# High parts of the MLP's weights cast on ScalarE, and the tail's constant products placed anew, in a kernel of attention and two mixtures

## The chip, the cores and the metric

One core of a Trainium2 chip runs the whole kernel. The metric is the device time of one execution in microseconds (us); lower is better. The result is compared with a reference in float32.

## The reference, cut to what matters

Three stages follow each other: causal attention with a decay (4 batches, 8 heads, 576 tokens, head size 64), an MLP with the gate h * sigmoid(1.702 h) (512 to 2048 to 512, on 2304 tokens), and a soft mixture of 8 experts over 32 slots.

```python
# attention
scores = scale * np.matmul(q, k.transpose(0, 1, 3, 2))
scores = np.where(causal, -1000000000.0, scores + decay)
attn = softmax(scores)                    # rows, with the maximum taken off
x = attn @ v                              # to (B*S, H*D)
# MLP
h = x @ w_in
x = (h * (1.0 / (1.0 + np.exp(-1.702 * h)))) @ w_out
# soft mixture
logits = x @ phi                          # 2304 x 32
d = exp(logits - logits.max(0)); d /= d.sum(0) + 1e-09
slot_input = d.T @ x                      # 32 x 512, over all tokens
slot_out[e] = np.maximum(slot_input[e] @ w1[e], 0.0) @ w2[e]
c = exp(logits - logits.max(1)); c /= c.sum(1) + 1e-09
out = c @ slot_out
```

## The kernel before, in words

Five engines run programs of their own that meet at semaphores: TensorE (PE) multiplies, VectorE (DVE), ScalarE (ACT) and GpSimd (POOL) move, split and scale, SyncE (SP) issues every DMA. Each runs its own instructions strictly in the order of the program text, so a wait holds back all that stands behind it on that engine.

**Split products.** A product of two float32 matrices is made of three faster ones: each operand is split into a high part (rounded to fp32r) and a low part (what is left), and PE multiplies high by high, high by low and low by high. For the MLP's weights, SP loads a piece of 128x512 into one of two slots of `stage` (`load_w`, L497), VectorE casts it into `wih` or `woh` (`w_split`, L790), and GpSimd subtracts the high part from the staged piece into `wil` or `wol` (L660). The next piece for that slot is loaded only when GpSimd has finished. There are 128 pieces: 4 batches, 4 quarters of the hidden size, 4 pieces of `w_in` and 4 of `w_out` each.

**Order.** `batch_steps` writes out one list of steps for each engine. Batch 0 of attention (to about 98 us) runs alone; then the heads of batches 1 to 3 are interleaved with the MLP of the batch before (to about 583 us), the MLP of the last batch runs alone (to about 696 us), and the tail with the experts follows. Batch 0's own four casts of the first quarter are steps of their own (`("split", t)`).

**MLP units.** An MLP of a batch has 64 units of 12 matmuls of 288 columns. In each quarter the first 8 units (kind 0) make hidden values: ScalarE takes the tanh out of PE's bank (`gate`, L729), VectorE makes `hid` from it and frees the bank (L921), ScalarE casts `hid` of the unit before to `gh` (L723), GpSimd makes `gl` (L643). The second 8 units (kind 1) multiply by `w_out`; VectorE adds the bank to `x2t` (L926, L928), ScalarE has no work but the last `gh`. PE alternates between two banks of `mb`, so a unit starts only when the bank of the unit before last has been read. VectorE's cast of piece t stands behind its own work of units 0, 1, 3 and 4 of a kind (`SPLIT_AT`): the pieces of `w_out` in kind 0, those of the next quarter's `w_in` in kind 1.

**A batch's last head.** The last head of a batch is finished in the next batch's first slot: ScalarE copies `olow` (L702), VectorE adds `xst` (L844), ScalarE casts `xh` (L706), VectorE subtracts `xl` (L849), and the next MLP may begin.

**Tail.** The logits of the last batch are turned (L1148, L1149), VectorE takes the maximum over tokens (`gmax`, L943), PE turns it (L1216), VectorE reduces it (`smax`) and makes a diagonal (`dmax`), PE spreads that to all partitions (L1220), VectorE subtracts it (`ew`, L950), ScalarE takes the exponential (L743), and PE sums tokens into slots (`dispatch`, L1231, 40 matmuls of 512 columns). `busy(n)` issues n matmuls of constants (L1159), whose results nobody reads. Then come the 8 experts. Their weights, 16 loads of 2 MB, go through a ring of ten buffers: the load of the tenth buffer (`ring_x`, L504) is issued when the dispatch is done (third count of `t_pe`), and the six loads that reuse a buffer when the expert before has been computed.

Of the kernel before, what the change touches and what calls it, by code (L numbers as in the profile page):

```python
# [53 lines left out]
SPLIT_AT = (0, 1, 3, 4)  # L54
# [12 lines left out]
TURN_AT = 6  # L67
SOFTMAX_AT = (8, 9, 10, 11, 18, 19, 20, 21)
SOFTMAX_EXP = 13
BUSY = (7, 16)  # L70
INV_SQRT_D = DIM ** -0.5
MASKED = 1e9
GATE = 1.702
# [159 lines left out]
def build(nc, q, k, v, f, w_in, w_out, phi, w1, w2, out):  # L233
    ctx = ExitStack()
    with ctx:
# [239 lines left out]
        def w_pieces(u, last):  # L475

            c, kind, j = unit_kind(u)
            if kind == 0:
                return c, 4, c
            if kind == 1 and not (last and c == QUARTERS - 1):  # L480
                return c + 1, 0, (c + 1) % QUARTERS
            return None
# [185 lines left out]
        def _(act):  # L668
            act.wait_ge(f_clip, 1)
            nc.scalar.activation(logf, f_sb, ACT.Ln).then_inc(f_log, 1)  # L670

            def step(b, m, st):
                if st[0] == "qk":
                    par = st[1] % 2
# [23 lines left out]
                elif st[0] == "pv":  # L698
                    s = st[1]
                    r0 = 64 * (s % 2)  # L700
                    act.wait_ge(attended, b * 8 + s + 1)
                    nc.scalar.copy(olow[r0:r0 + 64, :], pv_ps[64:P, :]).then_inc(o_low, 1)  # L702
                elif st[0] == "xsplit":
                    kt = st[1]
                    act.wait_ge(o_sum, m * 8 + 2 * kt + 2)
                    nc.scalar.copy(xh[:, kt, :], xst[:, kt, :]).then_inc(x_hi, 1)  # L706
                elif st[0] == "post":
                    for i in LAST_POST[st[1]]:
                        act.wait_ge(post_token, m * QT + i + 1)
                        nc.scalar.copy(x2last[0:QW[i], i, :], last_tokens[i][0:QW[i], :]).then_inc(token_out, 1)  # L710
                elif st[0] == "token":
                    i = st[1]
                    r = QW[i]
                    act.wait_ge(post_token, m * QT + i + 1)
                    nc.scalar.copy(x2tok[0:r, m * QT + i, :], bank_of("token", m, i)[0:r, :]).then_inc(token_out, 1)
                elif st[0] == "unit":
                    u = st[1]
                    c, kind, j = unit_kind(u)
                    k1 = m * 32 + 8 * c

                    def high(i):
                        act.wait_ge(unit_out, m * U_MLP + 16 * c + i + 3)
                        nc.scalar.copy(gh[:, i % FT, HALF * (i // FT):HALF * (i // FT + 1)],  # L723
                                       hid[:, i % RING, :]).then_inc(g_hi, 1)

                    if kind == 0:
                        act.wait_ge(unit_done, m * U_MLP + u + 1)
                        act.wait_ge(g_lo, k1 + j + 1)
                        nc.scalar.activation(gate[:, j % RING, :], bank_of("unit", m, u)[:, 0:HALF], ACT.Tanh,  # L729
                                             scale=GATE / 2).then_inc(h_tanh, 1)  # L730
                        if j:
                            high(j - 1)
                    elif j == 0:
                        high(7)
                    if m and u == SOFTMAX_EXP:
                        act.wait_ge(c_dve, (m - 1) * C_CHAIN + 2)
                        nc.scalar.activation(e5[:, :, :], e5[:, :, :], ACT.Exp).then_inc(c_exp, 1)
# [30 lines left out]
        def _(dve):  # L768
# [14 lines left out]
            dve.wait_ge(f_log, 1)  # L783
            dve.wait_ge(pads_made, 1)
            nc.vector.tensor_tensor_scan(cum, one_row, logf, 0.0, ALU.mult, ALU.add).then_inc(cum_made, 1)

            def w_split(order, which, t):
                hi = (wih, woh)[which]
                dve.wait_ge(w_dma[t % 2], 16 * ((order >> 1) + 1) if isinstance(order, int) else (order - t % 2) * 8 + 16)
                nc.vector.tensor_copy(hi[:, t, :], stage[:, t % 2, :]).then_inc(w_hi, 1)  # L790

            def step(b, m, st):
                if st[0] == "qk":
# [52 lines left out]
                elif st[0] == "xsplit":  # L846
# [1 line left out]
                    dve.wait_ge(x_hi, m * 4 + kt + 1)  # L848
                    nc.vector.tensor_tensor(xl[:, kt, :], xst[:, kt, :], xh[:, kt, :].bitcast(F32),  # L849
                                            ALU.subtract).then_inc(x_lo, 1)  # L850
                elif st[0] == "split":
                    w_split(st[1], 0, st[1])
                elif st[0] == "logits":
                    dve.wait_ge(post_logits, m + 1)
                    keep_turned(bank_of("logits", m, 0))
# [55 lines left out]
            def unit(b, m, u):  # L911
# [11 lines left out]
                else:  # L923
# [3 lines left out]
                    else:  # L927
                        nc.vector.scalar_tensor_tensor(out=dst, in0=bank[:, 0:HALF], scalar=0.5, in1=dst,  # L928
                                                       op0=ALU.mult, op1=ALU.add).then_inc(unit_out, 1)
                pieces = w_pieces(u, last)  # L930
                if pieces and j in SPLIT_AT:
                    t = SPLIT_AT.index(j)
                    w_split(m * 32 + 8 * pieces[0] + pieces[1] + t, pieces[1] // 4, t)
                if m and u in SOFTMAX_AT:
                    (keep_maxima, keep_values, token_max, token_sub, token_sum, token_eps, token_inv, token_weights
                     )[SOFTMAX_AT.index(u)](m - 1)
# [85 lines left out]
        def _(pe):  # L1022
# [188 lines left out]

            pe.wait_ge(lt_made, 1 + BATCH)
            turn_logits(last_turn)
            pe.wait_ge(t_dve, 1)
            pe.wait_ge(token_out, 1 + (BATCH - 1) * QT + 2)
            tr(zb[0:SLOTS, 0, 0:P], gmax[:, :], ident[:, :]).then_inc(t_pe, 1)  # L1216
            turn_last(4)
            busy(BUSY[0])
            pe.wait_ge(t_dve, 3)
            mm(zb[:, 1, 0:SLOTS], ones[0:SLOTS, :], dmax[:, :], start=True, stop=True).then_inc(t_pe, 1)  # L1220
            busy(BUSY[1])
            pe.wait_ge(t_act, 1)
            pe.wait_ge(t_dve, 4)
            pe.wait_ge(token_out, 1 + BATCH * QT)
# [107 lines left out]
```

## Time and profile before

| | us |
|---|---|
| median of 3 runs | 772.56 |
| lowest, highest | 771.88, 776.73 |
| the profiled execution's own time | 776.32 |
| its span, first to last instruction | 774.5 |
| PE busy | 718.1 |
| VectorE busy | 495.7 |
| GpSimd busy | 411.4 |
| ScalarE busy | 370.8 |

The profiled execution is 3.8 us longer than the median of the unprofiled runs, and lies near the highest of them. Its time is its span and 1.8 us around it. A busy time says how long an engine had an instruction in work; PE's matmuls overlap, so a busy PE isn't one at its peak. What counts for the time is where PE, the engine that is busy almost throughout, stood idle or ran at the lower clock.

### The profile page before, as it was taken

Reading aid. Unit: us, or ns where it says so; the run is one execution under the profiler, and the core shown is the slowest. Engines: PE = TensorE matmul, PEld = TensorE weight load, DVE = VectorE, ACT = ScalarE, POOL = GpSimd, SP = SyncE. Lnnn points to the kernel's source line nnn. Section 1 sums busy time; section 2 is a strip of 40 time slices with the busy share of each in tenths; the row PEclk is TensorE's granted clock in tenths of the full one; section 3 lists DMA queues with packets and bytes.
Section 4 is the critical chain, followed back from the end, with each engine's and each line's share of the span. In section 5 each row is a group of like instructions: output and inputs, shape, how many; then the busy total and the mean of one; then the engine's idle time right before and its main releaser. Section 6 shows DMA issues by size and latency. Waiting matters only on the chain.

```text
span 774.5 us, 15770 instructions
## 1 busy us (share of the span) xinstructions
PE 718.1 (93%) x6024; PEld 680.7 (88%) x6024; DVE 495.7 (64%) x1383; ACT 370.8 (48%) x903; POOL 411.4 (53%) x439
## 2 busy tenths in 40 slices
PE   3999979999999898999999989999999999998993
PEld 3888878999899898999999989999999999995562
DVE  5799857778877756786767667867553454424323
ACT  4777855464646464555556564646342133111113
POOL 4355356474757755565658554857385576530000
PEclk9899989999999999999999999999999999998998
DMA  4333322333333332233332423332213445498986
GB/s 102 105 91 105 94 63 80 94 82 91 94 93 94 93 81 74 84 98 90 94 99 52 119 54 93 94 93 79 64 48 114 158 133 194 140 396 300 385 332 244
DMA packets 96506, 96.65 MB, mean 125 GB/s; under 512 B 61296, under 2 KB 61296, under 8 KB 96432
## 3 DMA queue, kind: packets, MB, share of 16 engines
q1 hardware_dynamic: 96432, 95.66, 40.2%
q8 instruction: 48, 0.79, 0.4%
q14 instruction: 26, 0.21, 0.1%
HBM read 90.84 MB, written 4.79 MB: 123 GB/s over the span
## 4 chain that ended last, share of the span: by engine, by line
PE 69%; DVE 14%; ACT 5%; issue 3%; DMA 3%; POOL 2%; SPq 1%; DVEq 0%; POOLq 0%
PE mb L1204 47%; PE yb L1057 5%; PE zb L1076 5%; PE xb L1103 4%; DVE ptl L838 2%; DMA ring_b<-in_moe_w 2%; DVE prob L832 2%; ACT prob L684 2%; DVE kl L800 2%; DVE qs L796 2%; PE xb L1037 1%; POOL xl L633 1%; PE mb L1255 1%; DVE hid L921 1%; PE yb L1059 1%
## 5 line engine op out<-in xcount | busy, mean ns | idle before, releaser
L1204 PE MATMUL mb<-xh,wih 128*128 128x288 f32 x512 | 159.2, 311 | 11.0 <-DVE hid L921 5.2
L1204 PE MATMUL mb<-gh,woh 128*128 128x288 f32 x512 | 157.2, 307 | 4.2 <-DVE x2t L928 4.2
L1204 PE MATMUL mb<-xh,wil 128*128 128x288 f32 x512 | 151.9, 297 | 0.0
L1204 PE MATMUL mb<-xl,wih 128*128 128x288 f32 x512 | 151.9, 297 | 0.0
L1204 PE MATMUL mb<-gl,woh 128*128 128x288 f32 x512 | 151.0, 295 | 0.0
L1204 PE MATMUL mb<-gh,wol 128*128 128x288 f32 x512 | 150.9, 295 | 0.0
L643 POOL TENSOR_TENSOR gl<-hid,gh 128x288 fp32r<-128x288 f32 x128 | 114.4, 899 | 58.3 <-ACT gh L723 57.4
L684 ACT ACTIVATE prob<-prob,m_row 64x576 f32<-64x576 f32 (+4 forms) x160 | 96.4, 604 | 62.4 <-DVE m_row L818 61.9
L660 POOL TENSOR_TENSOR wol<-stage,woh 128x512 fp32r<-128x512 f32 x64 | 82.7, 1292 | 72.1 <-DVE woh L790 72.1
L660 POOL TENSOR_TENSOR wil<-stage,wih 128x512 fp32r<-128x512 f32 x64 | 83.1, 1300 | 71.4 <-DVE wih L790 71.4
L921 DVE SCALAR_TENSOR_TENSOR hid<-gate,mb 128x288 f32<-128x288 f32 x128 | 57.7, 451 | 98.8 <-ACT gate L729 97.3
L729 ACT ACTIVATE gate<-mb 128x288 f32<-128x288 f32 x128 | 52.6, 411 | 124.9 <-PE mb L1204 123.9
L1204 PEld LDWEIGHTS mb<-xh,wih 128*128 128x128 f32 x512 | 97.3, 190 | 14.5 <-DVE hid L921 7.6
L1204 PEld LDWEIGHTS mb<-gh,woh 128*128 128x128 f32 x512 | 96.6, 189 | 5.3 <-DVE x2t L928 5.3
L1204 PEld LDWEIGHTS mb<-xl,wih 128*128 128x128 f32 x512 | 97.4, 190 | 0.0
L1204 PEld LDWEIGHTS mb<-xh,wil 128*128 128x128 f32 x512 | 97.2, 190 | 0.0
L1204 PEld LDWEIGHTS mb<-gl,woh 128*128 128x128 f32 x512 | 96.6, 189 | 0.0
L1204 PEld LDWEIGHTS mb<-gh,wol 128*128 128x128 f32 x512 | 96.3, 188 | 0.0
L697 ACT CAST pth<-zb 128x512 fp32r<-128x512 f32 (+1 forms) x128 | 62.8, 491 | 69.6 <-PE zb L1076 69.0
L818 DVE CUSTOM_DVE_ANT_0 prob<-yb,cum_b 64x576 f32<-64x576 f32 (+4 forms) x160 | 83.5, 537 | 10.6 <-issue 10.4
L838 DVE TENSOR_TENSOR ptl<-zb,pth 128x512 fp32r<-128x512 f32 (+1 forms) x128 | 72.9, 569 | 11.5 <-ACT pth L697 10.8
L1076 PE MATMUL zb<-ident,prob 128*128 128x128 f32 x480 | 74.2, 279 | 3.5 <-DVE prob L832 3.1
(196 smaller groups left out, 1424.7 us busy)
## 6 DMA issues: line engine op xcount, KB each, us to landing
stage<-in_moe_w_in SPq DMA_DIRECT2D x64, 256.0 KB, 3.0
stage<-in_moe_w_out SPq DMA_DIRECT2D x64, 256.0 KB, 2.6
ring_a<-in_moe_w SPq DMA_DIRECT2D x16, 1024.0 KB, 7.3
ring_b<-in_moe_w SPq DMA_DIRECT2D x14, 1024.0 KB, 12.5
cum_b<-cum_dram SPq DMA_DIRECT2D x32, 288.0 KB, 3.7
qk_in<-in_q SPq DMA_DIRECT2D x32, 144.0 KB, 3.0
qk_in<-in_k SPq DMA_DIRECT2D x32, 144.0 KB, 3.4
v_in<-in_v SPq DMA_DIRECT2D x32, 128.0 KB, 3.2
```

The lines of the kernel that those rows point to most:

```text
L643: pool.tensor_tensor(gl[:, i % FT, HALF * (i // FT):HALF * (i // FT + 1)], hid[:, i % RING, :], gh[:, i % FT, HALF * (i // FT):HALF * (i / ...
L660: pool.tensor_tensor(lo[:, t, :], stage[:, t % 2, :], hi[:, t, :].bitcast(F32), ALU.subtract).then_inc(w_lo, 1)
L684: nc.scalar.activation(prob[0:r, par, POFF[i]:POFF[i] + w], prob[0:r, par, POFF[i]:POFF[i] + w], ACT.Exp, bias=m_row[0:r, par, i:i + 1], s ...
L697: nc.scalar.copy(pth[:, lo:hi], zb[:, c % 2, 0:hi - lo]).then_inc(p_hi, 1)
L729: nc.scalar.activation(gate[:, j % RING, :], bank_of("unit", m, u)[:, 0:HALF], ACT.Tanh, scale=GATE / 2).then_inc(h_tanh, 1)
L818: nc.vector.tensor_tensor_reduce(prob[0:r, par, o:o + w], ybf[0:r, base:base + w], cum_b[0:r, par, 0:w], 1.0, 3e38, ALU.add, ALU.min, m_ro ...
L838: nc.vector.tensor_tensor(ptl[:, lo:hi], zb[:, c % 2, 0:hi - lo], pth[:, lo:hi].bitcast(F32), ALU.subtract).then_inc(p_lo, 1)
L921: nc.vector.scalar_tensor_tensor(out=hid[:, j % RING, :], in0=gate[:, j % RING, :], scalar=1.0, in1=bank[:, 0:HALF], op0=ALU.add, op1=ALU. ...
L1057: mm(ybf[:, base + k0:base + k0 + kw], qs[:, par, P * i:P * i + P], x[:, par, k0:k0 + kw], start=not last, stop=last, skip_group_check=True)
L1076: ins = tr(zb[:, c % 2, at:at + P], prob[:, par, POFF[i] + P * kt:POFF[i] + P * kt + P], swapped if back else ident)
L1103: ins = mm(pv_ps[:, lo:q1], vs[:, par, kt, :], x[:, at:at + q1 - lo], start=(kt == 0 and x is pth), stop=(kt == (1 if q1 == 256 else 4) an ...
L1204: ins = mm(bank[:, 0:HALF], a[:, t, P * (j % 4):P * (j % 4) + P], x[:, t, cols], start=(i == 0), stop=(i == 11))
```

## The change

ScalarE issues all 128 casts of the weights' high parts. Its cast stands behind ScalarE's own work of the same unit (tanh and `gh` in kind 0; in kind 1 nothing but, in the first unit, the last `gh`). It waits for the same DMA; GpSimd waits for the same count as before, now raised by ScalarE. In kind 1 the cast no longer stands behind a wait for that unit's matmuls. The four casts of batch 0 move in the same way. In the tail the constant products are 9, 3 and 14 in place of 7 and 16: 9 between the turning of the logits and the turning of `gmax`, 3 (7 before) ahead of the spreading of the maximum, 14 (16 before) ahead of the dispatch.

```diff
-BUSY = (7, 16)
+BUSY = (9, 3, 14)
@@ scalar
+            def w_split(order, which, t):
+                hi = (wih, woh)[which]
+                act.wait_ge(w_dma[t % 2], 16 * ((order >> 1) + 1) if isinstance(order, int) else (order - t % 2) * 8 + 16)
+                nc.scalar.copy(hi[:, t, :], stage[:, t % 2, :]).then_inc(w_hi, 1)
+
@@ scalar, step
+                elif st[0] == "split":
+                    w_split(st[1], 0, st[1])
@@ scalar, unit, behind tanh and gh
+                    pieces = w_pieces(u, is_last(m))
+                    if pieces and j in SPLIT_AT:
+                        t = SPLIT_AT.index(j)
+                        w_split(m * 32 + 8 * pieces[0] + pieces[1] + t, pieces[1] // 4, t)
@@ vector
-            def w_split(order, which, t):
-                hi = (wih, woh)[which]
-                dve.wait_ge(w_dma[t % 2], 16 * ((order >> 1) + 1) if isinstance(order, int) else (order - t % 2) * 8 + 16)
-                nc.vector.tensor_copy(hi[:, t, :], stage[:, t % 2, :]).then_inc(w_hi, 1)
-                elif st[0] == "split":
-                    w_split(st[1], 0, st[1])
@@ vector, unit, behind hid or x2t
-                pieces = w_pieces(u, last)
-                if pieces and j in SPLIT_AT:
-                    t = SPLIT_AT.index(j)
-                    w_split(m * 32 + 8 * pieces[0] + pieces[1] + t, pieces[1] // 4, t)
@@ tensor, tail
             turn_logits(last_turn)
+            busy(BUSY[0])
             pe.wait_ge(t_dve, 1)
             pe.wait_ge(token_out, 1 + (BATCH - 1) * QT + 2)
             tr(zb[0:SLOTS, 0, 0:P], gmax[:, :], ident[:, :]).then_inc(t_pe, 1)
             turn_last(4)
-            busy(BUSY[0])
+            busy(BUSY[1])
             pe.wait_ge(t_dve, 3)
             mm(zb[:, 1, 0:SLOTS], ones[0:SLOTS, :], dmax[:, :], start=True, stop=True).then_inc(t_pe, 1)
-            busy(BUSY[1])
+            busy(BUSY[2])
             pe.wait_ge(t_act, 1)
```

## Rows read from the trace of the kernel before

**Rows 1.** The page's part 1: busy time of each engine and its share.
```profile
PE 718.1 (93%) x6024; PEld 680.7 (88%) x6024; DVE 495.7 (64%) x1383; ACT 370.8 (48%) x903; POOL 411.4 (53%) x439
```

**Rows 2.** Windows, attention with MLP: stretch, length, busy PE, PEld, DVE, ACT, POOL, clock, DMA.
```profile
300.00:400.00 100.00, 99.30 (x771) 98.42 (x770) 72.01 (x206) 51.76 (x128) 59.72 (x63) 1.00 0.33 91
```

**Rows 3.** Waits of PE from 100 to 600 us: total us, times, longest.
```profile
PE mb L1204 <- DVE x2t L928: 5.6, 6, 1.5
PE mb L1204 <- DVE hid L921: 5.2, 7, 1.8
```

**Rows 4.** Tile view of wih: ns least, median, most; VectorE's waits before.
```profile
L790 DVE CAST wih<-stage x64: 405/427/1468, 43.3 to 665.6; 128x512 fp32r<-128x512 f32 x64
  DMA stage<-in_moe_w_in: 13.5, 12
```

**Rows 5.** ScalarE's casts from memory to memory, by line.
```profile
L723 ACT CAST gh<-hid x128: 417/426/442, 109.7 to 682.6; 128x288 fp32r<-128x288 f32 x128
L706 ACT CAST xh<-xst x16: 655/672/687, 97.2 to 577.1; 128x576 fp32r<-128x576 f32 x16
```

**Rows 6.** Timeline around 120 us: start, length, instruction, idle time before it.
```profile
118.37 1.43 DVE L790 CAST woh<-stage 128x512 fp32r<-128x512 f32 x1
...
124.43 0.41 PE L1204 MATMUL mb<-xh,wih 128*128 128x288 f32 x1 [1.83 <-DVE hid L921]
```

**Rows 7.** Windows: the stretch behind that wait.
```profile
124.40:130.00 5.60, 5.57 (x31) 5.55 (x32) 0.86 (x3) 2.83 (x7) 2.08 (x3) 0.70 0.44 108
```

**Rows 8.** Timeline around 256 us, where a batch's last head is finished.
```profile
253.99 0.64 ACT L702 COPY olow<-xb 64x576 f32<-64x576 f32 x1
...
257.98 0.40 PE L1204 MATMUL mb<-gh,woh 128*128 128x288 f32 x1 [1.49 <-DVE x2t L928]
```

**Rows 9.** Timeline from 262 to 271 us.
```profile
262.60 0.43 DVE L790 CAST wih<-stage 128x512 fp32r<-128x512 f32 x1 [2.28 <-DMA stage<-in_moe_w_in]
264.88 1.13 DVE L790 CAST wih<-stage 128x512 fp32r<-128x512 f32 x1 [0.89 <-DMA stage<-in_moe_w_in]
...
266.67 0.72 ACT L684 ACTIVATE prob<-prob,m_row 128x512 f32<-128x512 f32 x1 [5.67 <-DVE m_row L818]
...
271.02 0.40 PE L1204 MATMUL mb<-xh,wih 128*128 128x288 f32 x1 [1.34 <-DVE x2t L928]
```

**Rows 10.** Timeline of ScalarE: a slot of batch 0, and a unit of the last MLP.
```profile
52.08 0.59 ACT L697 CAST pth<-zb 128x512 fp32r<-128x512 f32 x1 [0.40 <-PE zb L1076]
...
654.59 0.41 ACT L729 ACTIVATE gate<-mb 128x288 f32<-128x288 f32 x1 [0.87 <-PE mb L1204]
```

**Rows 11.** Timeline of the tail, from the turning of gmax to the tenth load.
```profile
700.67 0.28 PE L1216 MATMUL zb<-ident,gmax 128*32 128x128 f32 x1 [1.48 <-DVE gmax L943]
...
701.15 0.98 PE L1159 MATMUL mb<-ident_r 128*128 128x128 f32 x7
...
702.06 0.42 PE L1220 MATMUL zb<-dmax,ones 32*128 32x32 f32 x2
...
702.41 3.67 PE L1159 MATMUL mb<-ident_r 128*128 128x128 f32 x16
...
703.37 0.74 ACT L743 ACTIVATE ew<-ew 128x640 f32<-128x640 f32 x1 [1.36 <-DVE ew L950]
...
706.02 4.73 PE L1231 MATMUL xb<-x2tok,ew 128*32 128x512 f32 x27
...
712.11 0.92 SPq L504 DMA_DIRECT2D ring_x<-in_moe_w  x2
```

**Rows 12.** Windows of the tail: fillers, dispatch, its end, the experts.
```profile
702.00:704.00 2.00, 2.00 (x12) 1.88 (x10) 1.61 (x6) 0.64 (x2) 0.00 (x0) 0.58 1.00 385
708.00:710.00 2.00, 2.00 (x16) 0.44 (x12) 0.00 (x0) 0.00 (x0) 0.00 (x0) 0.72 0.81 332
709.50:713.50 4.00, 2.85 (x26) 0.78 (x18) 1.04 (x3) 0.00 (x0) 0.00 (x0) 1.00 0.13 27
713.50:750.00 36.50, 34.67 (x687) 21.16 (x687) 12.81 (x44) 4.29 (x13) 0.00 (x0) 0.95 1.01 389
```

## The prediction, made before the changed kernel was run

> **What bounds the kernel now.** I read the page's part 1 first: PE is busy for 718.1 of 774.5 us, VectorE for 64% and ScalarE for 48% [rows 1]. Then the windows by stage, to see whether that holds in each. Where attention and MLP run together it does: between 300 and 400 us PE is busy for 99.30 us of 100 at the full clock, VectorE for 72.01 and ScalarE for 51.76 [rows 2]. So most of the span is PE's own work, and no other engine's busy time is worth anything there. What can be won stands in PE's waits. From 100 to 600 us those that end with VectorE's release of a bank sum to 5.6 and 5.2 us, in 6 and 7 places [rows 3]. This is the ceiling for the first part of the change: 10.8 us, and a little more where a wait also lowered the clock. Last I read the tail in order of time, since the second part acts there. PE waits 1.48 us for the maximum [rows 11], the clock falls within the next stretch (0.58 from 702 to 704, 0.72 from 708 to 710) [rows 12], and the dispatch starts at 706.02, though its exponential had ended at 703.37 + 0.74 = 704.11 [rows 11].
>
> **Part one, what leaves VectorE.** 128 casts go. The median of 427 ns is the cast's own time, and the longest, 1468 ns, three times that, has a wait in it [rows 4]. At 0.43 us each at least, VectorE loses 55 us of work, and about 11 us of each 100 in the mixed stretch. It also loses its waits for the weights' DMA, 13.5 us in 12 places [rows 4], which held back its own reading of PE's banks.
>
> **What comes to ScalarE.** No row has a ScalarE cast of 128x512 from SBUF. The neighbours are 426 ns for 288 columns and 672 ns for 576 [rows 5], both within 3% from least to most. On the line through them 512 columns take 426 + 224 x 0.854 = 617 ns; the ends are 587 (the 128x512 copy out of PSUM, 0.59 us [rows 10]) and 672. With 0.62 us, 128 casts are 79 us, and ScalarE goes from 371 to about 450 us busy, and from 52 to about 65 of each 100 in the mixed stretch. It stays below VectorE's present load.
>
> ScalarE's rule in the Trainium skill, "ScalarE: Activation LUTs", section "Rules for kernel authors", speaks against the change: plain elementwise work belongs on VectorE, which is quicker per element. The rows agree on the price of one cast, 0.62 against 0.43 us. By the rule the kernel would lose that difference 128 times, 24 us; the sum here charges it only where a queue behind it is late.
>
> Against this stands "SBUF — State Buffer", section "SBUF: two separate sides": VectorE's two-port operations and GpSimd's operations lock each other out of one pair of ports, and ScalarE has its own. The stretch from 427 to 1468 ns agrees with it, and by it the casts on ScalarE would all be alike.
>
> **Where it lies beside other work.** In the MLP that runs alone ScalarE idles 0.87 us before each tanh [rows 10], and the cast needs 0.62. It fits, so the beat of the units stays; if it did not, the tanh would be late by the excess. In kind 1 ScalarE has nothing at all to do for the MLP. What is queued behind a cast that waits for its DMA is ScalarE's attention work: the copies `pth`, and the exponentials, for which VectorE's `ptl` and PE's transposes wait. At 262.60 the wait was 2.28 us on VectorE; ScalarE was idle 5.67 us up to 266.67, waiting for VectorE [rows 9]. There the wait only changes from a busy engine to an idle one. GpSimd, which waits for each cast, gets it 0.2 us later where ScalarE starts at VectorE's time, and sooner in kind 1, where ScalarE doesn't wait for matmuls; with GpSimd SP's queue moves, whose next load waits for it. PE needs all four pieces only at the next kind, some three units later.
>
> **Term by term, for the profiled execution.**
> 1. At 271.02 PE waited 1.34 us for `x2t`. VectorE had been late since 262.60: 2.28 us of waiting and a cast, then 0.89 us and a cast of 1.13 [rows 9]. More than 1.34 us of this goes: -1.3 us. The third batch's end, where the same wait precedes a shorter one, gives another -0.4.
> 2. At 124.43 PE waited 1.83 us for `hid`. VectorE's chain ahead of it holds the cast of 1.43 us at 118.37 [rows 6], but what followed the cast waited for ScalarE's last exponential, and this comes 0.6 us later when casts stand before it. I take half: -0.7 us.
> 3. Five shorter waits of 0.4 to 0.9 us for `hid`, a little each: -0.4 us.
> 4. In batch 0, four slots carry a cast on VectorE, which has hardly a gap there. On ScalarE it stands ahead of a `pth` with 0.40 us of idle time before it [rows 10], so 0.2 us of it shows and 0.4 goes from VectorE: 4 x -0.15 = -0.6 us.
> 5. Where a batch's last head is finished, the cast lands ahead of `olow` at 253.99, and `olow`, `xst`, `xh`, `xl` and `x2t` follow each other to PE's wait of 1.49 us at 257.98 [rows 8]. All of this comes later by the cast, less its overlap: +0.5 us, at two of three places, and +0.2 at the third, where `olow` has idle time before it.
>
> Sum: -1.3 - 0.4 - 0.7 - 0.4 - 0.6 + 1.2 = -2.2 us. From both sides: all of PE's waits for VectorE in [rows 3] go at best, though I find no reason for more than half, -5; at worst the five gains are nothing and term 5 also costs clock, +4.
>
> **Part two, the tail.** The 9 products take 9 x 0.12 = 1.1 us, by the 7 that took 0.98 [rows 11]. They lie within PE's 1.48 us of waiting and cost nothing; without that cover they would cost the 1.1. The 3 in place of 7 end 0.46 us sooner; `dmax` was ready by then, so the spreading of the maximum, `ew` and the exponential come 0.4 us sooner (VectorE's memset in between keeps the rest). The exponential then ends at 703.7. The 14 start at 701.95 and take 1.7 us at the full clock, so they end at 703.65. The dispatch starts at 703.8 in place of 706.02: -2.2 us. The 16 took 3.67 us, that is at the half clock [rows 11]. The dispatch itself ran from 706.02 to about 709.1 at half the clock (0.72 from 708 to 710 is 0.28/0.5 x 2 = 1.1 us of it there) [rows 12]; at full clock these 3.1 us are 1.55. Together -3.8 us, if the clock holds.
>
> Does it reach the end? The tenth load is issued at 712.11, right behind the dispatch [rows 11], and the DMA engines moved almost nothing from 709.5 to 713.5 (share 0.13), then ran full to 750 (1.01) [rows 12]. The end of the tail is these transfers' end. An issue 3.8 us sooner closes a gap of 4.0 x 0.87 = 3.5 us and little is lost of it: I take -3.5. Beyond it nothing more comes, since the transfers before the gap aren't sooner.
>
> If the clock falls all the same, the chain is 0.4 us sooner and two products fewer run at the half clock; the dispatch starts at about 704.7 and does a longer part at the half clock: it ends 0.8 us sooner.
>
> **Against the median.** The profiled execution is 776.32; 776.32 - 2.2 - 3.5 = 770.6. The median is 3.8 us lower. A tail in which the clock had held before would explain 3.1 of that: the 16 products would have ended at 704.4, and the dispatch at 708.9. Then the second part wins 0.6 us, and 772.56 - 2.2 - 0.6 = 769.8. Both ways meet near 770.2, which I predict.
>
> **The rivals.**
> - *The casts move nothing* (0.2). PE waits at 13 places in 500 us, and each wait has other causes in its chain. For it: term 2's chain passes through ScalarE too. Against it: term 1's delay is VectorE's alone. Time: 772.56 - 0.6 = 772.0.
> - *The clock falls in the tail again* (0.2). For it: in [rows 11, 12] a stretch that was filled with such products from end to end, 702.41 to 706, did not bring the clock back. Against it: PE's largest gap there shrinks from 1.48 to 0.4 us. Time: 776.32 - 2.2 - 0.8 = 773.3.
> - *The last heads' chain costs the clock: slower* (0.15). At 122.6 PE stood for 1.83 us and the clock then fell (0.70 from 124.4 to 130 [rows 7], that is 0.30/0.5 x 5.6 = 3.4 us at the half clock and half of it lost, 1.7). At 257.98 it stood for 1.49 and the clock held. If term 5 makes 2.0 of it, it may fall there, three times over: 3 x 1.7 + 1.2 = 6.3 us, less the other terms' 3.4 and the tail's 0.6: 772.56 + 2.3 = 774.9. It decides from a wait between 1.5 and 1.8 us on.
> - *ScalarE becomes late throughout* (0.05). Should each cast of the mixed stretch delay a tanh that PE waits for by 0.1 us, 90 casts are 9 us: 780. The 0.87 us of [rows 10] speak against it.
>
> In "TensorE: Matmul & The Clock Gate", section "HAM oscillation — how this bites in real kernels", the Trainium skill also ties the fall to idle stretches of PE; the trace agrees, with the two waits just named.
>
> **How the numbers follow.** The forecast holds with 0.4, at 770.2, and ends within 768 and 772.5. The range that leaves out no more than 2 in 10 reaches from -5 in the first part, 767.0, to the slower rival, 775.0. A measurement of this kernel can tell about 1% from no change, 7.7 us. Faster than 764.8 takes more than all bounds together: 0.04. Slower than 780.3 needs the last rival: 0.04. Within 1%: 0.92.
>
> **What would show it.** Casts of 0.60 to 0.65 us on ScalarE, alike from first to last; VectorE at about 430 us busy, ScalarE at about 450. PE's wait near 271 gone; the waits near 258 and 421 longer by half a microsecond. In the tail: clock 1.00 from 702 to 708, dispatch from about 3 us behind the turning of `gmax`, no gap in the DMA. I'm wrong if PE's waits are put down to ScalarE's tanh, if casts on ScalarE vary as they did on VectorE, or if the DMA was not what set the end.

## The result, and the profile after

| | before | after |
|---|---|---|
| median, us | 772.62 | 764.12 |
| the profiled execution's own time | 776.32 | 763.06 |
| its span | 774.5 | 761.3 |

The ratio is 0.9875, with a 95% interval of 0.983 to 0.9919: the changed kernel is 1.25% faster. In a second measurement (e0, below) it took 763.56 us against 774.34, a ratio of 0.9855 (0.983 to 0.988). A few executions took far longer (3907.29 us, one of after); the ratios leave them out and the medians don't, and without them those of after, e1 and e12 are 763.79, 767.55 and 762.24. The prediction was 770.2, in a range from 767.0 to 775.0: the time lies 2.9 us below the range, and "within 1%" was wrong as well, though the first interval alone, 0.8% to 1.7%, would leave it open.

First the busy times, part 1 of the page of after, beside [rows 1], and the window of the mixed stretch beside [rows 2].

```profile
PE 711.8 (94%) x6027; PEld 677.7 (89%) x6027; DVE 444.2 (58%) x1255; ACT 436.6 (57%) x1031; POOL 399.2 (52%) x439
```

```profile
300.00:400.00 100.00, 100.00 (x775) 99.18 (x774) 65.08 (x187) 64.68 (x156) 59.58 (x65) 1.00 0.35 100
```

VectorE has lost 51.5 us and ScalarE gained 65.8; they now carry the same load. PE did 775 matmuls in these 100 us, where it did 771. Next the tile view of `wih` in after (nanoseconds least, median, most), which answers to [rows 4].

```profile
L675 ACT CAST wih<-stage x64: 602/618/628, 41.4 to 655.4; 128x512 fp32r<-128x512 f32 x64
```

On ScalarE the cast takes 618 ns at the median and 628 at most. On VectorE it took 427, and 1468 at most; the view by lines gives the mean, which the prediction didn't read:

```profile
L790 DVE CAST wih<-stage 128x512 fp32r<-128x512 f32 x64 | 34.5, 539 | 13.6 <-DMA stage<-in_moe_w_in 13.5
L790 DVE CAST woh<-stage 128x512 fp32r<-128x512 f32 x64 | 33.7, 527 | 0.6 <-DMA stage<-in_moe_w_out 0.6
```

So the casts that left VectorE sum to 68.2 us, record by record, with 14.2 us of waiting. VectorE's records overlap one another, and its busy time fell by 51.5. Now PE's waits from 100 to 600 us in after (total us, times, longest), beside [rows 3].

```profile
PE mb L1204 <- DVE xl L855: 4.3, 1, 4.3
PE mb L1204 <- DVE hid L925: 3.2, 6, 1.4
PE mb L1204 <- DVE x2t L932: 3.2, 3, 1.4
...
PE xb L1037 <- issue: 1.0, 1, 1.0
```

The two groups of [rows 3] fell from 5.6 and 5.2 to 3.2 each, 4.4 us together. The last line was 2.5 us in 3 places before and is 1.0 in one. Two of these three waits of before, by its timeline:

```profile
330.37 0.69 PE L1037 MATMUL xb<-ident,qk_in 96*128 96x96 f32 x6 [0.70 <-issue]
...
492.86 0.69 PE L1037 MATMUL xb<-ident,qk_in 96*128 96x96 f32 x6 [0.74 <-issue]
```

**Where the 13.3 us went.** Each of the 256 MLP units begins with the same matmul, so the start of each unit in after can be set against the same unit in before. The offset grows at these places:

| stretch of before, us | what changed there | us |
|---|---|---|
| to 106 | half clock for 7 us at 20 to 27 in before only (-0.8; chance, see below), batch 0's casts (-0.55) | -1.4 |
| 106 to 133 | the wait for `hid` at 124, 1.83 to 1.39; the half clock behind it (-1.6); an earlier end of the half clock around the first unit (-0.4; chance, see below) | -2.4 |
| 133 to 288 | waits of 0.48 (199) and 1.34 (271) gone, 0.88 (292) to 0.34 | -2.3 |
| 320 to 354 | the wait at 330, "issue", gone | -0.7 |
| 422 to 454 | the wait for `hid` at 454, 0.87 to 0.34 | -0.4 |
| 454 to 517 | the wait at 492, "issue", gone | -0.8 |
| 558 to 589 | waits of 0.39 for `ptl` and 0.44 for `x2t` gone, and smaller ones | -1.3 |
| elsewhere | | -0.2 |
| **to the logits** | | **-9.5** |
| **the tail**, from the turning of `gmax` to the end: 73.86 to 70.06 | | **-3.8** |

The stretch at 20 to 27 us is in batch 0, ahead of all that was changed; e7, e10 and e15, whose casts are on ScalarE, show it too, in whole or in part, so it isn't the change's. Nor are the 0.4 us behind the first unit: e1, e8 and e9, whose code is that of after up to the logits, don't have them. This is the grain of these offsets: at the last unit those five profiles (after, e0, e1, e8, e9) stand 9.5, 9.7, 8.8, 8.6 and 7.8 us ahead of before. A difference of one microsecond between two profiles says nothing. In the timeline of after PE's wait at the place of [rows 6], and at that of [rows 8]:

```profile
122.22 0.40 PE L1204 MATMUL mb<-xh,wih 128*128 128x288 f32 x1 [1.39 <-DVE hid L925]
```

```profile
249.59 0.62 ACT L675 CAST wih<-stage 128x512 fp32r<-128x512 f32 x1
250.23 0.64 ACT L707 COPY olow<-xb 64x576 f32<-64x576 f32 x1
...
252.38 0.76 DVE L855 TENSOR_TENSOR xl<-xst,xh 128x576 fp32r<-128x576 f32 x1 [0.74 <-ACT xh L713]
...
253.57 0.40 PE L1204 MATMUL mb<-gh,woh 128*128 128x288 f32 x1 [1.36 <-DVE x2t L932]
```

And the tail of after, beside [rows 11] (timelines of PE, of ScalarE and of SP's queue) and [rows 12] (windows):

```profile
691.23 0.28 PE L1217 MATMUL zb<-ident,gmax 128*32 128x128 f32 x1 [0.54 <-DVE gmax L943]
...
692.16 0.40 PE L1221 MATMUL zb<-dmax,ones 32*128 32x32 f32 x2
692.50 1.78 PE L1159 MATMUL mb<-ident_r 128*128 128x128 f32 x14
694.40 3.20 PE L1232 MATMUL xb<-x2tok,ew 128*32 128x512 f32 x27
```

```profile
693.61 0.74 ACT L754 ACTIVATE ew<-ew 128x640 f32<-128x640 f32 x1 [1.04 <-DVE ew L950]
```

```profile
698.96 0.92 SPq L504 DMA_DIRECT2D ring_x<-in_moe_w  x2
```

```profile
694.00:701.00 7.00, 5.64 (x50) 2.18 (x49) 3.85 (x11) 0.68 (x2) 0.00 (x0) 1.00 0.99 385
```

Counted from the turning of `gmax`, the dispatch starts at 3.17 us (5.35 before), the tenth load is issued at 7.73 (11.44 before), the clock is 1.00, and the DMA share is 0.99 where [rows 12] had 0.13.

### The profile page after: what moved, and what is told of

Same layout as the page of the kernel before. It is cut to its first block, busy times and chain, and to the rows that moved or that the text cites. A ratio compares the mean times of both kernels' runs of the same rounds, so it can differ in the third digit from the quotient of the medians.

```text
span 761.3 us, 15776 instructions
## 1 busy us (share of the span) xinstructions
PE 711.8 (94%) x6027; PEld 677.7 (89%) x6027; DVE 444.2 (58%) x1255; ACT 436.6 (57%) x1031; POOL 399.2 (52%) x439
## 4 chain that ended last, share of the span: by engine, by line
PE 77%; DVE 9%; ACT 7%; DMA 3%; issue 2%; POOL 0%; SPq 0%; DVEq 0%; POOLq 0%
PE mb L1204 52%; PE yb L1057 6%; PE zb L1076 5%; PE xb L1103 5%; DMA ring_b<-in_moe_w 2%; PE xb L1037 2%; ACT prob L689 2%; DVE ptl L844 1%; DVE prob L838 1%; ACT xh L713 1%; PE mb L1256 1%; PE yb L1059 1%; DVE kl L806 1%; DVE qs L802 1%; PE yb L1295 1%
## 5 line engine op out<-in xcount | busy, mean ns | idle before, releaser
L643 POOL TENSOR_TENSOR gl<-hid,gh 128x288 fp32r<-128x288 f32 x128 | 105.2, 827 | 74.6 <-ACT gh L730 72.9
L736 ACT ACTIVATE gate<-mb 128x288 f32<-128x288 f32 x128 | 52.5, 410 | 81.8 <-PE mb L1204 81.4
L932 DVE SCALAR_TENSOR_TENSOR x2t<-mb,x2t 128x288 f32<-128x288 f32 x96 | 43.4, 455 | 71.0 <-PE mb L1204 70.9
```

The costliest lines, as they stand in the source:

```text
L643: pool.tensor_tensor(gl[:, i % FT, HALF * (i // FT):HALF * (i // FT + 1)], hid[:, i % RING, :], gh[:, i % FT, HALF * (i // FT):HALF * (i / ...
```

## The experiments

Where a number is given "at the logits", it is the offset of the last MLP unit of the profiled execution. "After" is the changed kernel. The medians of before beside the four sets of runs are 774.36 (e1 to e4), 774.16 (e5 to e7, e11), 774.34 (e0, e8 to e10) and 774.01 (e12 to e15). The first two sets ran on chips of their own, so their medians go beside the 763.56 of e0 only through the ratios.

### The two parts alone

```diff
 e1_casts_only, against after
-BUSY = (9, 3, 14)
+BUSY = (0, 7, 16)
 e2_busy_only, against before: BUSY = (9, 3, 14), with busy(9) behind turn_logits
```

> The change's first part alone: ScalarE casts, and the tail's constant products stand as before (0, 7 and 16). Theory A, VectorE's lateness: VectorE was late at about ten places where PE waited for it, two of which the profile put to 'issue', and the casts alone win about 7 us of the 8.5, so 765.5. Theory B, the tail: the casts win the 2.2 us of the sum on record and the rest came from the tail, so about 770.

> The second part alone: VectorE casts, products 9, 3 and 14. Theory A: 0.6 us where the clock would have held anyway and up to 3.5 where not, so a median of 770 to 772. Theory B: 766 to 767.

Measured: e1 767.88 us, ratio 0.9914 (0.988 to 0.9948); e2 773.64, 0.999 (0.997 to 1.001). At the logits e1 stands 8.84 us ahead of before, e2 0.35. So the gain of the main phase is the casts'. In the tail of e1 the clock falls, as it did before, and the sixteen products take 3.13 us:

```profile
691.84 0.29 PE L1217 MATMUL zb<-ident,gmax 128*32 128x128 f32 x1 [1.48 <-DVE gmax L943]
...
693.56 3.13 PE L1159 MATMUL mb<-ident_r 128*128 128x128 f32 x16
```

The parts don't add up in the medians: the constants alone win 0.7 us, on top of the casts about 4 (767.88 to 763.56, on two chips).

### Half of the casts each

```diff
 e3_wih_on_act: ScalarE casts w_in's pieces (kind 1), VectorE those of w_out
-                    if pieces and j in SPLIT_AT:
+                    if pieces and j in SPLIT_AT and kind == 1:
 e4_woh_on_act: the reverse (kind == 0 on ScalarE; batch 0's four on ScalarE in both)
```

> As the changed kernel, but the pieces of w_out (kind 0, between tanh and hid) are cast on VectorE as before; only those of w_in, in whose units ScalarE has nothing to do, are cast on ScalarE. Theory A1, what counts is VectorE standing in front of a late DMA (all such waits but 0.6 us were before pieces of w_in): nearly all of the gain stays, about 765. Theory A2, what counts is VectorE's load in kind 0, where its casts met GpSimd: half of it or more goes, 768 to 770.

> The counterpart: only the pieces of w_out are cast on ScalarE, those of w_in (with the waits for a late DMA) on VectorE. Theory A1: little gain is left beside the tail's, 770 to 771. Theory A2: most of it, 765 to 767.

Measured: e3 769.67 us, 0.9947 (0.9929 to 0.9965); e4 768.28, 0.9928 (0.99 to 0.9956). At the logits they are 3.4 and 5.1 us ahead of before, together 8.5 (batch 0's four casts, 0.55 us, are in both), near e1's 8.84. VectorE's waits of 13.6 us for the DMA all lie with `w_in`, whose casts give 3.4 us; `w_out`'s, with 0.6 us of waiting, give 5.1. By the medians, whose intervals overlap, the two are not told apart. So a late weight is at most a part of what made VectorE late. PE's waits divide as the casts do: e3 waits 3.2 us for `x2t` and 5.2 for `hid`, e4 5.1 and 3.2. What `w_out` has beyond `w_in` in these profiles is seen in the windows behind the wait at 124 us, of e3 and of e4:

```profile
124.00:130.00 6.00, 6.00 (x35) 5.93 (x36) 1.26 (x4) 3.30 (x9) 2.83 (x4) 0.72 0.39 96
```

```profile
124.00:130.00 6.00, 6.00 (x48) 5.91 (x47) 2.86 (x6) 2.94 (x8) 3.31 (x4) 1.00 0.37 91
```

With the `w_out` casts on VectorE the wait is 1.82 us (1.80 to 1.83 in all four such profiles) and the clock falls to half behind it (0.72); with them on ScalarE it is 1.39 and the clock stays (1.00). This held in every profile that is read: the clock fell there in before, e2, e3 and e13, and in none of the thirteen with the `w_out` casts on ScalarE (eleven with a wait of 1.4 us, e5 and e11 with 1.6).

### VectorE given back the time, without the work

```diff
 e5_dve_copy, behind VectorE's hid or x2t at the 124 former places (no result is read; the lines of gap's semaphore are left out)
+                if w_pieces(u, last) and j in SPLIT_AT:
+                    nc.vector.tensor_copy(gap[:, :], gap[:, :])      # 256 columns
 e6_dve_memset: nc.vector.memset(gap[:, :], 0.0) in its place; e14_dve_two_memsets: two of them
```

> The changed kernel, and VectorE again does a copy where its cast stood (256 columns in place, about 0.3 us, behind hid or x2t of units 0, 1, 3 and 4), which waits for no DMA and which nobody reads. Theory L (load): VectorE's time in these places is what made PE wait, so a good part of the gain goes: of 6.5 us some 3 to 4, that is 767 to 768 where the changed kernel has 764. Theory D (the late DMA behind which VectorE stood, 13.5 us of waits): the gain stays but for 1 us, 764 to 765.

> As the run with the copy, but a memset of 256 columns of SBUF, which reads nothing. If VectorE's copies were long because they waited for GpSimd (longest 1468 ns against a median of 427), a memset should wait less: 1 to 2 us faster than with the copy. If only the length of the instruction counts, the two are within 1 us.

> The changed kernel with two memsets of 0.27 us at VectorE's places of the casts, 0.54 us in all: as long as the copies of the earlier run were on average (0.55), but reading nothing. If only the time that VectorE is kept counts, the loss is that of the copies, 6 to 7 us, 770 to 771. If it is the meeting with GpSimd, when one has to wait for the other, 2 to 4 us, 766 to 768.

The tile views of `gap`, of e5 and of e6:

```profile
L940 DVE COPY gap<-gap x124: 273/418/1416, 106.1 to 676.2; 128x256 f32<-128x256 f32 x124
```

```profile
L940 DVE MEMSET gap<- x124: 272/272/272, 106.0 to 671.4; 128x256 f32 x124
```

| kernel | from start to end, per place on VectorE, mean | loss at the logits against after | median | ratio (95%) |
|---|---|---|---|---|
| after (e0_after) | 0 | 0 | 763.56 | 0.9855 (0.983 to 0.988) |
| e6, memset | 0.27 us | 3.1 | 766.10 | 0.9889 (0.9865 to 0.9912) |
| e14, two memsets | 0.66 us, both | 9.6 | 772.18 | 0.9974 (0.9962 to 0.9986) |
| e5, copy | 0.55 us | 8.0 | 771.27 | 0.9956 (0.9939 to 0.9973) |
| before, the cast (with e2: 0.53 us) | 0.53 us | 9.1 (e2) | 774.34 | 1 |

The second memset of e14 waits for the first, so the two take 0.66 us from start to end and not 0.54:

```profile
115.48 0.66 DVE L941 MEMSET gap<- 128x256 f32 x2
```

Nothing waits for `gap`, no DMA feeds it, and ScalarE still makes all casts. Yet 0.55 us of it takes back 8.0 us at the logits. What counted was VectorE's time at these places. It needn't come from GpSimd: the memset is 272 ns each time, and two of them cost at least as much as the copy. And the mean seems to count, not the median: a straight line between the two kernels with memsets gives 7.8 us for the copy's mean of 0.55 and 5.6 for its median of 0.42 (an estimate), where 8.0 was measured.

It seems not to be in proportion. The single memset has 0.41 of the pair's time and 0.3 of its loss (3.1 of 9.6 at the logits, 2.5 of 8.6 in the medians). But its own price isn't settled: its interval overlaps that of after, and 1.1 of its 3.1 us come from one wait of PE, 0.9 us for `wil` at 610, behind a cast on ScalarE that waited for its DMA. e7 has that wait too, without a memset.

### Does ScalarE's freedom from the unit's matmuls matter, and has ScalarE room?

```diff
 e7_act_waits_unit: the cast of kind 1 waits for its unit again
+                        if kind:
+                            act.wait_ge(unit_done, m * U_MLP + u + 1)
 e11_act_double: behind each of ScalarE's 128 casts one more copy, unread (256 columns)
+                nc.scalar.copy(gap[:, :], gap[:, :])
```

> The changed kernel, but ScalarE's cast of a piece of w_in waits for the matmuls of its unit, as VectorE's did by its place behind x2t. If the casts gain by standing free of that wait (the next load and GpSimd come sooner, and olow isn't held up), 1 to 2 us slower than the changed kernel, with the wait near 253 us longer. If not, the same within 0.5 us.

> The changed kernel, and ScalarE does one more copy behind each cast (256 columns, about 0.4 us, 128 times, which nobody reads). Theory S (slack): ScalarE, at 65 us of 100, has room for 51 us more, and the time grows by less than 2 us. The rival by which ScalarE becomes late: each 0.4 us shows at a tanh or at olow now and then, 5 us or more.

e7: 764.56 us, 0.9866 (0.9842 to 0.989), against 0.9855 for after. The freedom is worth nothing that can be told. e11: 772.81, 0.9977 (0.9958 to 0.9997); the copy takes 404 ns at the median. ScalarE has no slack either: 0.40 us more, 128 times, takes back 8.3 us at the logits. PE's waits of e11 from 100 to 600 us:

```profile
PE mb L1210 <- DVE x2t L938: 5.4, 4, 2.1
...
PE mb L1210 <- DVE hid L931: 4.1, 8, 1.6
```

And where a batch's last head is finished, the wait and the half clock behind it:

```profile
255.45 0.40 PE L1210 MATMUL mb<-gh,woh 128*128 128x288 f32 x1 [1.90 <-DVE x2t L938]
...
256.31 0.44 PE L1210 MATMUL mb<-gh,wol 128*128 128x288 f32 x1
```

That is the prediction's slower rival: at 1.36 us the clock held there, at 1.90 and 2.06 (the next batch's) it fell. It came with 0.40 us more per cast than the change has. The two stretches at the half clock, 3.4 us each, explain 3.4 of the 8.3 us; most of the rest is longer waits.

### The tail's three numbers

```diff
 e9_busy_0_3_14, against after
-BUSY = (9, 3, 14)
+BUSY = (0, 3, 14)
 e8_busy_9_7_16: BUSY = (9, 7, 16);  e0_after: the changed kernel again, on their chip
```

> The changed kernel without the nine products behind the turning of the logits (0, 3, 14). If these keep the clock up: the half clock comes back in the profile's first stretches of the tail and the median is 1 to 3 us above the changed kernel's. If the gain of the tail comes from the shorter rows (3 and 14), within 0.5 us of it.

> The counterpart: the nine are kept, the others are as before (9, 7, 16). If the nine alone keep the clock, the dispatch ends 0.6 us later than in the changed kernel, since dmax and the exponential wait for the products, and the median is within 0.7 us of it.

> The changed kernel again, beside the runs below on one chip: 0.9875 of the kernel before, 764 us where that has 773.

| from the turning of `gmax`, us | dispatch starts | next product behind it | last expert's last product starts | end |
|---|---|---|---|---|
| before | 5.35 | 11.30 | 52.8 | 73.9 |
| e1 (0, 7, 16) | 4.78 | 11.37 | 53.0 | 73.9 |
| e9 (0, 3, 14) | 4.12 | 10.69 | 52.5 | 73.5 |
| e8 (9, 7, 16) | 3.65 | 8.07 | 49.6 | 71.1 |
| after (9, 3, 14) | 3.17 | 7.60 | 48.7 | 70.1 |
| e0 (9, 3, 14) | 3.17 | 7.60 | 48.8 | 69.8 |

The medians: e9 766.74 us (0.9897, 0.9874 to 0.992), e8 765.72 (0.9884, 0.9859 to 0.9909), e0 763.56 (0.9855). Without the nine the wait for the maximum is 1.48 us again and the half clock is back; the nine keep the clock and are worth 3.2 us. Fourteen products that follow such a wait without a pause take 2.92 us (1.78 in after):

```profile
694.15 2.92 PE L1159 MATMUL mb<-ident_r 128*128 128x128 f32 x14
```

The 3 and 14 in place of 7 and 16 are worth 0.47 us at the dispatch, and 2.2 us in the medians, where at most 0.7 was expected. The intervals overlap, though each of e8's four executions (764.99 and more) is longer than each of e0's (763.82 and less).

### The longest wait left: ahead of the first unit

After has one wait of 4.28 us, for `xl`, ahead of the first MLP unit; of the ten microseconds from 96 to 106, (1 - 0.67)/0.5 x 10 = 6.6 are at the half clock (window below). The same remedy as in the tail:

```diff
 e10_fill_first, ahead of the first unit of the first MLP
+                            if isinstance(m, int) and m == 0:
+                                busy(34)
```

> A try at a faster version: the changed kernel, and PE issues 34 constant products before the MLP's first unit, where it waits 4.3 us for the low part of the last piece of x at 101 us and then runs 6.8 us at the half clock. If the wait is what costs the clock, the half clock behind it goes, and with it 3.4 us: 760.5. If the products end behind the wait, or the clock falls all the same: 0 to 1 us slower.

> The control for it on the same chip: the version with the 34 products alone, 0.983 of the kernel before, 762.

```profile
96.30 3.99 PE L1159 MATMUL mb<-ident_r 128*128 128x128 f32 x34
100.86 0.40 PE L1206 MATMUL mb<-xh,wih 128*128 128x288 f32 x1 [0.58 <-DVE xl L855]
```

The window from 96 to 106 us of after, then of e10:

```profile
96.00:106.00 10.00, 5.34 (x24) 4.99 (x24) 4.26 (x9) 5.44 (x11) 4.42 (x4) 0.67 0.26 61
```

```profile
96.00:106.00 10.00, 9.42 (x77) 9.20 (x77) 4.57 (x9) 6.22 (x13) 6.33 (x6) 1.00 0.21 48
```

The clock holds (1.00 for 0.67). At the logits e10 is 2.7 us ahead of after and e15, the same kernel measured again, 1.2; their batch 0 differs by chance. Counted from the first unit on, both are 2.1 to 2.2 us ahead. Medians: e10 761.84 us, 0.9833 (0.9809 to 0.9858); e15 762.48, 0.9861 (0.9844 to 0.9879). With e12, which has the same 34 products, these are the lowest medians of the study, and the best version found; beside after (763.56) the gain of 1.1 to 1.7 us is less than the intervals can settle, and the profiles alone show its mechanism.

### Does a second fall behind the dispatch explain the rest?

In seven of the profiles so far (e2, e3, e4, e6, e7, e10, e11) the clock falls once more, for 3.4 us, 10 to 12 us behind the turning of `gmax`. Before has such a fall too, at 15.3 us, as its dispatch ends later. PE has waited for `part` just before (1.24 us, in after too, where the clock holds). In e2 `gmax` is turned at 700.34; its window:

```profile
711.00:715.00 4.00, 3.50 (x33) 1.19 (x34) 0.88 (x4) 0.38 (x1) 0.00 (x0) 0.57 1.00 333
```

```diff
 e12_fill_both: e10, and 9 and 3 products of constants behind the dispatch and behind `part`
 e13_busy_post: the same 9 and 3 on top of e2
+            for _ in range(9):
+                mm(zb[:, 1, 0:P], ident_r[:, :], ident_r[:, :], start=True, stop=True)
```

> The version with 34 products before the first unit, and 9 and 3 more behind the dispatch, where PE waits 1.2 us for part and 0.4 us for slot_t. If the half clock about 9 us behind the turning of gmax comes from that idle stretch, and delays the loads that wait for the first expert: it goes, and the tail ends 1.5 to 2.5 us sooner, 760 where the version without them has 762. If the tail's spread comes from the DMA itself: no change.

> Casts on VectorE, products 9, 3 and 14, and the 9 and 3 behind the dispatch. The tail's change alone gained only 0.8 us where it gains 3 to 4 beside the other part. If that was the second fall of the clock: 771 to 772. If the gain is lost for another reason: 773.6 again.

e12: 763.23 us, 0.9851 (0.9836 to 0.9866), beside e15's 0.9861 on the same chip: no gain. No profile of it is read, but the mean clock that each execution was granted is on record: 0.994 to 0.995 in its three fastest, 0.989 to 0.992 in e15's five. So they ran at the half clock for less time, and were no faster (761.34 to 762.36 us beside 761.86 to 765.65). e13: 772.76, 0.9988 (0.9976 to 1.0), beside 0.999 for e2: no gain. In the profile of e13 the fall is there all the same, so it tests the remedy and not the suspect. That the second fall makes the constants worth less in e2 is not shown; e12 speaks against it, and so does before, whose tail from the first expert on is no longer than that of after (59.5 us, 59.4) in spite of the fall.

## Why the prediction failed, point by point

**The bound was found where it was, and its size was wrong.** PE's waits for VectorE were indeed what could be won. The ceiling of 10.8 us in [rows 3] was not exceeded by the waits themselves (4.4 us of it went). But the sum of -2.2 us became -9.5, or -8.3 without the two chance shares (0.8 and 0.4). Five steps failed: the half clock behind the wait at 124 was no term, "a little each" was no working, term 5 had the wrong sign, PE's waits put down to "issue" were left out, and part two was costed as if it were worth the same beside part one as alone.

- *What leaves VectorE.* "At 0.43 us each at least" took the median for the price, where the view by lines had a mean of 0.53. The size came out near all the same: VectorE's busy time fell by 51.5 us, where 55 was said, and stands at 444 ("about 430" doesn't follow from 495.7 - 55). ScalarE stands at 437, where 450 was said. So this was not the step that failed. What failed is that no term asked what this time is worth to PE: e5 and e14 show 7.7 and 8.6 us of kernel time for 0.55 and 0.66 us at 124 places.
- *Term 1* (-1.3 and -0.4): the wait of 1.34 us at 271 is gone, as predicted; at the third batch's end the wait of 0.44 is gone, as predicted, and with it one of 0.39 for `ptl` that was no term. The reason given, a late weight, holds at 271 and fails as a general one (e3 against e4).
- *Term 2* (-0.7): the wait went from 1.83 to 1.39, -0.44. The step that failed is the one not written: the half clock of [rows 7] was named in a rival, with its price of 1.7 us (1.6 by the offsets), and was not taken as something that could be won. The rival even said that it "decides from a wait between 1.5 and 1.8 us on", and half of term 2 took the wait below that. This and term 5 are the largest errors of part one. (The bound between 1.5 and 1.8 is of these places alone: in the tail, in [rows 11], 1.48 us was followed by the fall.)
- *Term 3* (-0.4): 0.48 to 0, 0.88 to 0.34 and 0.87 to 0.34 are 1.6 us. "A little each" was not worked out. At these places VectorE had a cast ahead of `hid`, and what a cast takes, 0.54 us, is what each lost.
- *Term 4* (-0.6): measured -0.55. Right.
- *Term 5* (+1.2): wrong in sign. The waits at the three last heads went from 1.49 to 1.36, 1.49 to 1.35 and 0.66 to 0.47, -0.5 together. `olow` does come behind a cast on ScalarE. But in before VectorE's `xl` took 1.40 us, and the same instruction takes 0.76 in after. In before GpSimd was at its own three `xl` until 256.94, and VectorE's, started at 256.15, ended 0.6 us after that; in after GpSimd's three had ended at 252.48, only 0.10 us behind the start of VectorE's. The Trainium skill has a rule for this: by "SBUF — State Buffer", section "Who interferes with whom", a VectorE instruction with two inputs in SBUF contends with a GpSimd instruction that reads SBUF. The rows agree: GpSimd's `gl` behind its `xl` then took 1.37 us beside VectorE's, where its median is 0.81. The step that failed is that the chain was costed by its first instruction alone; the lengths of its last were taken as fixed (the first row is of after, the last of before):

```profile
248.28 4.20 POOL L633 TENSOR_TENSOR xl<-xst,xh 128x576 fp32r<-128x576 f32 x3 [1.70 <-ACT xh L713]
...
256.15 1.40 DVE L849 TENSOR_TENSOR xl<-xst,xh 128x576 fp32r<-128x576 f32 x1 [0.74 <-ACT xh L706]
```

- *Missing:* the waits marked "issue" at 330 and 492 us, 1.44 us. The prediction filtered PE's waits by "<- DVE". That they vanish with VectorE's casts, and with `w_out`'s alone (e4 has 1.0 in 1 place, e3 2.4 in 3), shows that they came of VectorE's time, though the profile names no releaser.
- *The bounds.* "I find no reason for more than half, -5" was an absence of working, not a bound. With the clock's 1.7 and the "issue" waits' 1.4 the honest lower end was -8 or so.

**Part two.** The working for the profiled execution was right step by step: the start of the dispatch was to come 2.2 us sooner and came 2.18 sooner (5.35 to 3.17), its end 3.8 and 3.7, the end of the kernel 3.5 and 3.8, and the gap in the DMA is closed. The rival that the clock falls again did not come true with the nine; e9 shows what it would have been. What failed is the step to the median, where 0.6 us was taken for the constants. For the constants alone this is what was measured (e2: 0.7). Beside the casts they are worth more, 3.2 us by e9 and about 4 by e1, and no sentence of the prediction asked whether the two parts act on each other. The granted clock of every execution shows where the difference lies. Its median is 0.985 in before and 0.985 in e2: with the casts on VectorE the constants save no clock that can be seen. With the casts on ScalarE it is 0.986 and 0.9865 without the nine (e1, e9), and 0.991, 0.9905 and 0.9875 with them (after, e0, e8), with three to six executions each. As half of the time at the half clock is lost, 0.004 of 763 us is about 3 us (an estimate). So what the constants add beside the casts is clock; why they add none without them stays open. Whether before's tail kept its clock in the unprofiled executions, as the prediction assumed, can't be told from a mean: their 0.985 is above the profiled one's 0.978, but of that the chance stretch at 20 us alone is 0.004.

**A rule of the Trainium skill.** "ScalarE: Activation LUTs", section "Rules for kernel authors", in the Trainium skill would have simple elementwise work (it lists relu, max, min, add and mul) on VectorE, since it is quicker per element. For these casts VectorE is, by 0.19 us at the median and 0.09 at the mean. Here the rule, taken as the measure, points the wrong way: the kernel gains 6.5 us by the slower engine (e1), as the quicker one was the one PE waited for. In the Trainium skill, "SBUF — State Buffer", section "Who interferes with whom", also says that VectorE's copies and casts can take a pair of ports that GpSimd needs, and that instructions with at most one input in SBUF outside the two-port modes do not. The traces agree: of e5's copies the 105 that began while GpSimd was at work took 273 to 1416 ns, 600 in the mean, and the other 19 took 276 to 289. The memset of e6 is 272 each time, and the casts on ScalarE are within 602 to 635.

**What stays open.** Why the constants win 0.7 us alone and 3 to 4 on top of the casts. In all profiles with (9, 3, 14) the tail is alike to within 0.2 us until the first expert's first product, 10.7 us behind the turning of `gmax`; from there it takes 59.1 to 59.8 us in after, e0, e5 and e15, which have no second fall, and 59.6 (e6), 60.2 to 61.0 (e13, e2, e7, e10, e14, e11), 61.7 (e4) and 62.6 (e3) where it is there. In the nine with a second fall the DMA moved less for a few us: 288 to 357 GB/s from 20.7 to 24.7 us behind `gmax`, where the four others have 398 to 406. Windows of e2 and e10, which start 20.7 and 21.5 us behind `gmax`, then of after, 19.8 behind:

```profile
721.00:725.00 4.00, 3.83 (x91) 2.71 (x84) 1.96 (x8) 0.65 (x2) 0.00 (x0) 1.00 1.00 314
```

```profile
710.00:714.00 4.00, 3.83 (x92) 2.89 (x92) 2.36 (x8) 0.65 (x2) 0.00 (x0) 1.00 0.89 323
```

```profile
711.00:715.00 4.00, 3.83 (x92) 2.86 (x92) 2.36 (x8) 0.65 (x2) 0.00 (x0) 1.00 1.03 402
```

Before, with its fall at 15.3 us, takes 59.5, so the fall alone doesn't bring the loss. Whether the clock or the DMA comes first, and what sets 314 or 402 GB/s, was not found.

## What to carry to other kernels

Before costing work that leaves an engine, ask what each microsecond of that engine's lateness costs the one that sets the end; measure it by adding an unread instruction at the place: here 0.55 us at 124 places cost 7.7 us, and 0.66 us cost 8.6. Count every wait of the bounding engine near those places, the ones put down to "issue" too, and for each the half clock behind it: a wait shortened from 1.83 to 1.39 us won 0.44 and 1.6 more. Where two parts of a change are costed apart, ask also what each is worth beside the other. Where the bounding engine must wait, put constant products into the wait and not behind it.

## What the runs showed of the hardware

- At one place the length of PE's wait went with the half clock behind it, and across places the same length didn't. At 124 us a wait of 1.80 to 1.83 us was followed by the half clock in four profiles of four, 1.4 in none of eleven and 1.6 in neither of two. At the last heads 1.17 to 1.49 weren't, 1.90 and 2.06 were. In the tail 1.48 was, and 0.54 wasn't.
- Products of constants behind such a wait don't save the clock (14 in 2.92 us, 16 in 3.13 and 3.67); products in the wait do (9 in the tail, 34 in 3.99 us at 96 us).
- VectorE's copy from SBUF to SBUF takes up to five times its time (273 to 1416 ns) beside GpSimd, and the memset of the same size doesn't (272). For the kernel the mean of the copies counted, 0.55 us, and not their median, by the estimate made with the memsets.
- ScalarE's cast of 128x512 from SBUF to SBUF, fp32 to fp32r, takes 618 ns at the median in after; the estimate by the line through [rows 5] was 617.
